# Causal mixing and two gated layers on one core: another fixed order of the engines, and transposes from a doubled copy

## What is computed

```python
w = softmax of weight_gen over its last axis (7 taps, for 8 groups of 24 columns)
out = np.einsum('bshk,bskhg->bshg', w, x_unf)          # causal mixing, 7 taps
x = out.reshape(B * S, 192)
gate = 1.0 / (1.0 + np.exp(-(x @ w_gate)))             # w_gate, w_val: 192 x 1536
y = (gate * (x @ w_val)) @ w_out                       # 1536 x 192
h = y @ w_in                                           # 192 x 2048
P = a[0] + a[1] * h + a[2] * h * h + a[3] * h**3
Q = 1.0 + abs(b[0]) * abs(h) + abs(b[1]) * h * h
out = (P / (Q + 1e-06)) @ w_out2                       # 2048 x 192
```

## Time and profile before

| | |
|---|---|
| median of 3 runs | 1507.46 us (1506.63 to 1507.68) |
| the profiled execution, its own time | 1503.02 us |
| its span | 1501.2 us |
| TensorE clock granted, mean | 0.987 |
| PE matmuls | 7168, busy 93% of the span |
| DVE | busy 86% |
| ACT | busy 70% |
| GpSimd | busy 28% |

### The profile page before, as it was taken

How to read it: one execution, slowest core, us unless ns; L and a number is a source line. 1 busy time by engine, 2 the same in 40 slices (tenths; PEclk the granted TensorE clock), 3 DMA queues, 4 the chain that set the end, 5 groups by cost and what they waited for, 6 DMA issues and landing times.

```text
span 1501.2 us, 18228 instructions
## 1 busy us (share of the span) xinstructions
PE 1402.0 (93%) x7168; PEld 1235.1 (82%) x7168; DVE 1292.8 (86%) x1327; ACT 1044.0 (70%) x1325; POOL 424.9 (28%) x204
## 2 busy tenths in 40 slices
PE   2789999999999999999999999999999999999876
PEld 1678888898888888888888888888888888888766
DVE  6547988989888898988989898898988889888898
ACT  2437777786776777677677767767677777777774
POOL 0650704306060340705125070421607033000000
PEclk9899999999999999999999999999999999999998
DMA  9410000000000000000000000000000000000000
GB/s 198 117 73 30 0 31 11 30 11 30 11 1 30 12 30 11 30 12 1 30 11 30 11 16 15 11 31 12 30 12 0 30 11 1 11 1 11 1 11 11
DMA packets 13102, 36.22 MB, mean 24 GB/s; under 512 B 1240, under 2 KB 6872, under 8 KB 12760
## 3 DMA queue, kind: packets, MB, share of 16 engines
q1 hardware_dynamic: 12952, 35.05, 7.8%
q0 software_dynamic: 64, 0.00, 0.0%
...
## 4 chain that ended last, share of the span: by engine, by line
PE 51%; DVE 33%; ACT 10%; issue 6%; DMA 1%; DVEq 0%; SPq 0%; ACTq 0%
PE ring L280 28%; PE acc L308 21%; DVE work L592 8%; DVE work L604 7%; DVE work L597 4%; ACT work L428 4%; DVE work L578 3%; DVE work L582 3%; DVE work L587 3%; ACT work L423 2%; DVE u L573 2%; ACT L423 1%; ACT work L418 1%; PE ring L335 1%; DVE xt L558 1%
## 5 line engine op out<-in xcount | busy, mean ns | idle before, releaser
L308 PE MATMUL acc<-out_w,work 128*128 128x192 f32 x2048 | 383.7, 331 | 23.1 <-DVE work L604 23.1
L308 PEld LDWEIGHTS acc<-out_w,work 128*128 128x128 f32 x2048 | 347.3, 193 | 43.8 <-DVE work L604 30.4
L280 PE MATMUL ring<-yt,in_w 128*128 128x512 f32 x1280 | 367.9, 417 | 3.1 <-DVE yt L567 3.1
L413 ACT ACTIVATE work<-ring,coef 128x512 f32<-128x512 f32 x256 | 175.0, 683 | 237.9 <-PE ring L280 168.3
L308 PE MATMUL acc<-out_w,u 128*128 128x192 f32 x1536 | 282.3, 327 | 12.6 <-DVE u L573 12.6
L280 PE MATMUL ring<-xt,gate_w 128*128 128x512 f32 x960 | 272.5, 414 | 18.4 <-DVE work L582 13.8
L308 PEld LDWEIGHTS acc<-out_w,u 128*128 128x128 f32 x1536 | 260.3, 190 | 30.2 <-DVE u L573 13.9
L578 DVE TENSOR_TENSOR work<-ring,work 128x512 f32<-128x512 f32 x256 | 175.5, 685 | 126.3 <-ACT work L418 125.8
L280 PEld LDWEIGHTS ring<-yt,in_w 128*128 128x128 f32 x1280 | 236.6, 190 | 42.8 <-issue 3.3
L280 PE MATMUL ring<-xt,val_w 128*128 128x512 f32 x960 | 256.4, 397 | 0.0
L505 POOL TENSOR_TENSOR mixed<-window,mixw 128x768 f32<-128x768 f32 x14 | 21.7, 1550 | 776.0 <-PE ring L340 776.0
...
## 6 DMA issues: line engine op xcount, KB each, us to landing
...
```

What stands on the lines that cost most here:

```text
L280: last = nc.tensor.matmul(dst[:, :], wt[:, c], xs[:, :], start=n == 0, stop=n == 4)
L308: last = nc.tensor.matmul(dst, src[:, n * P:(n + 1) * P], w[:, i, :], start=i == 0 and n % 2 == 0, stop=i == last_i and n % 2 == 1, skip_g ...
L413: nc.scalar.activation(den(n), h[:, :], ACT.Abs, scale=coef[:, 6:7])
```

## The change

- **Transposes.** `mixed` and `ysb` get 256 columns for each 128 tokens, the last 64 a copy of columns 128 to 191. ACT writes it: x_twice is one more copy for each tile (PE now waits for it by s_twice), y_copy becomes two copies. The second bank is then four transposes of columns 128 to 255 in place of eight (L341 of the kernel after). The mixing instructions are the same in number and size, with views of more dimensions.
- **Weights.** The lower 64 rows of each first weight had a high copy in both halves of one tile and a low copy in both halves of another. Now one tile holds the high part in rows 0 to 63 and the low part in rows 64 to 127, and is used for two matmuls in a row, against the high part of x in both halves (xt 2) and the low part in both halves (a fourth tile, xt 3). The number of matmuls of a product stays five. x_low and y_low write 128 rows in place of 64 for their second part, and the split of such a weight's piece writes its low part in 64 rows in place of 128.
- **Order.** PE, ACT and DVE have new orders within a quarter. The lags are the same: B_LAG = 8 counts blocks where 2 counted quarters. X and Y are units of the string. NK is 73, and the last two quarters hold nothing. h_parts and linear are one function, hidden.

The diff, cut to its core (besides it, functions return at once for blocks that don't exist, and mix has views for the wider `mixed`):

```diff
-QUARTER = "21b" "2a1b" "2ab1" "2ab"
+
+
+QUARTER = "12a212abbbXbYa12"
 A_LAG = 1
-X_AT = 10
-Y_AT = 8
+B_LAG = 8
 OFF2 = 5
-B_LAG = 2
...
-        gate_w = [sb(f"gate_w{n}", [P, F1 * P], F32R) for n in range(4)]
-        val_w = [sb(f"val_w{n}", [P, F1 * P], F32R) for n in range(4)]
-        in_w = [sb(f"in_w{n}", [P, F2 * P], F32R) for n in range(4)]
+        gate_w = [sb(f"gate_w{n}", [P, F1 * P], F32R) for n in range(3)]
+        val_w = [sb(f"val_w{n}", [P, F1 * P], F32R) for n in range(3)]
+        in_w = [sb(f"in_w{n}", [P, F2 * P], F32R) for n in range(3)]
...
-        mixed = sb("mixed", [P, J, D])
+        mixed = sb("mixed", [P, J, 2 * P])
...
-        xt = [[sb(f"xt{b}_{n}", [P, T], F32R) for n in range(3)] for b in range(2)]
-        yt = [[sb(f"yt{b}_{n}", [P, T], F32R) for n in range(3)] for b in range(2)]
-        ysb = sb("ysb", [P, J, D])
...
+        xt = [[sb(f"xt{b}_{n}", [P, T], F32R) for n in range(4)] for b in range(2)]
+        yt = [[sb(f"yt{b}_{n}", [P, T], F32R) for n in range(4)] for b in range(2)]
+        ysb = sb("ysb", [P, J, 2 * P])
...
-                passes = [(w[0], src[0]), (w[1], src[0]), (w[0], src[1]), (w[2], src[2]), (w[3], src[2])]
+                passes = [(w[0], src[0]), (w[1], src[0]), (w[0], src[1]), (w[2], src[2]), (w[2], src[3])]
...
-                    dst = bank(u, j, 1)
-                    nc.tensor.transpose(dst[:, n * P:(n + 1) * P], src[:, n, D - P:D], ident[:, :])
-                    last = nc.tensor.transpose(dst[0:DB, n * P:(n + 1) * P], src[:, n, DA:D], ident[:, :])
+                    last = nc.tensor.transpose(bank(u, j, 1)[:, n * P:(n + 1) * P], src[:, n, DA:2 * P], ident[:, :])
                 return last
 
             def x_transposes(j):
-                pe.wait_ge(s_mix, MIXES * (j + 1))
+                pe.wait_ge(s_twice, j + 1)
...
-                m, a, n, b = 3 * k, 3 * k - A_LAG, 4 * (k - OFF2), 4 * (k - OFF2 - B_LAG)
-                for at, u in enumerate(QUARTER):
+                m, a, n, b = 3 * k, 3 * k - A_LAG, 4 * (k - OFF2), 4 * (k - OFF2) - B_LAG
...
+            def x_twice(j):
+                if not 0 <= j < NCH:
+                    return
+                act.wait_ge(s_mix, MIXES * (j + 1))
+                nc.scalar.copy(mixed[:, :, D:2 * P], mixed[:, :, DA:D]).then_inc(s_twice, 1)
...
-                nc.scalar.copy(ysb[:, :, :].rearrange("p (a n) d -> p a (n d)", a=2),
-                               acc1[:, :, 0:2 * D]).then_inc(s_ysb, 1)
+                src = acc1[:, :, 0:2 * D].rearrange("p a (n d) -> p a n d", d=D)
+                dst = ysb[:, :, :].rearrange("p (a n) d -> p a n d", a=2)
+                nc.scalar.copy(dst[:, :, :, 0:D], src)
+                nc.scalar.copy(dst[:, :, :, D:2 * P], src[:, :, :, DA:D]).then_inc(s_ysb, 1)
...
-                one, m = k < 4 * NCH, 3 * k
-                two, n = 0 <= k - OFF2 < 4 * NCH, 4 * (k - OFF2)
-                if two:
-                    h_parts(n)
-                    linear(n)
-                if one:
-                    sigmoid(m)
+                m, n, q = 3 * k, 4 * (k - OFF2), k - OFF2
+                sigmoid(m)
                 if k == 0:
                     split_high(4)
                     split_high(5)
                     exponential(1)
                     split_high(6)
                     split_high(7)
-                if 0 < k < 4 * NCH + 1 and k % 4 == 0:
+                hidden(n)
+                if k % 4 == 0:
                     y_copy(k // 4 - 1)
-                if two:
-                    h_parts(n + 1)
-                    linear(n + 1)
-                if one:
-                    sigmoid(m + 1)
+                if k % 4 == 2:
+                    x_twice((k + 1) // 4 + 1)
+                hidden(n + 1)
+                sigmoid(m + 1)
                 if k == 1:
                     exponential(2)
                 if k in (2, 3):
-                    for p in range(3 * k + 2, 3 * k + 5):
-                        split_high(p)
-                if 0 <= k - OFF2 - 1 < 4 * NCH:
-                    rsqrt(k - OFF2 - 1)
-                if two:
-                    h_parts(n + 2)
-                    linear(n + 2)
-                if 0 < k < 4 * NCH + 1 and k % 4 == 0:
+                    for c in range(3 * k + 2, 3 * k + 5):
+                        split_high(c)
+                rsqrt(q - 1)
+                hidden(n + 2)
+                rsqrt_squared(q - 1)
+                if k % 4 == 3:
+                    x_high(k // 4 + 1)
+                if k % 4 == 0:
                     y_high(k // 4 - 1)
-                if 0 <= k - OFF2 - 1 < 4 * NCH:
-                    rsqrt_squared(k - OFF2 - 1)
-                if one:
-                    sigmoid(m + 2)
-                if k % 4 == 3 and k // 4 + 1 < NCH:
-                    x_high(k // 4 + 1)
-                if two:
-                    h_parts(n + 3)
-                    linear(n + 3)
-                if k >= OFF2 + B_LAG + 3 and (k - OFF2 - B_LAG) % 4 == 3:
-                    z_copy((k - OFF2 - B_LAG) // 4)
+                sigmoid(m + 2)
+                hidden(n + 3)
+                if (k - OFF2) % 4 == 1:
+                    z_copy((k - OFF2 - 1) // 4 - 1)
...
-                nc.vector.tensor_tensor(lo[:, at:at + size], piece[n % BUFFERS][:, 0:size],
-                                        hi[:, at:at + size].bitcast(F32), ALU.subtract).then_inc(s_split, 1)
+                nc.vector.tensor_tensor(lo[rows, at:at + size], piece[n % BUFFERS][rows, 0:size],
+                                        hi[rows, at:at + size].bitcast(F32), ALU.subtract).then_inc(s_split, 1)
...
-                nc.vector.tensor_tensor(dst[2][DB:P, :], bank("X", j, 1)[DB:P, :], dst[2][DB:P, :].bitcast(F32),
+                nc.vector.tensor_tensor(dst[3][:, :], bank("X", j, 1)[:, :], dst[2][:, :].bitcast(F32),
...
-                one, m = k < 4 * NCH, 3 * k
-                two, n = 0 <= k - OFF2 < 4 * NCH, 4 * (k - OFF2)
-
-                p = n // 2 - 2
-                late, due = 0 <= p - 1 < N2 // 2, 0 <= p < N2 // 2
-                if two:
-                    quadratic(n)
-                    cubic(n)
-                if one:
-                    gated(m)
+                m, n, p = 3 * k, 4 * (k - OFF2), 2 * (k - OFF2)
+                gated(m)
                 if k == 0:
                     split_low(4)
                     split_low(5)
@@ -632,46 +657,37 @@
                         soft(step)
                     split_low(6)
                     split_low(7)
-                if late:
-                    reciprocal(p - 1)
-                    quotient(p - 1)
-                if two:
-                    quadratic(n + 1)
-                    cubic(n + 1)
-                    denominator(n // 2)
-                if one:
-                    gated(m + 1)
+                quadratic(n)
+                cubic(n)
+                reciprocal(p - 3)
+                denominator(p - 1)
+                quotient(p - 3)
+                gated(m + 1)
                 if k == 1:
-                    soft(12)
-                    soft(13)
-                    soft(14)
+                    for step in range(12, 15):
+                        soft(step)
                 if k == 2:
-                    soft(15)
-                    soft(16)
-                    soft(17)
+                    for step in range(15, 18):
+                        soft(step)
                 if k in (2, 3):
                     for c in range(3 * k + 2, 3 * k + 5):
                         split_low(c)
-                if two:
-                    quadratic(n + 2)
-                    cubic(n + 2)
-                if 0 < k < 4 * NCH + 1 and k % 4 == 0:
+                quadratic(n + 1)
+                denominator(p)
+                cubic(n + 1)
+                quadratic(n + 2)
+                cubic(n + 2)
+                newton_product(p - 2)
+                if k % 4 == 0:
                     y_low(k // 4 - 1)
-                if due:
-                    newton_product(p)
-                    reciprocal(p)
-                if one:
-                    gated(m + 2)
-                if due:
-                    quotient(p)
-                if k % 4 == 3 and k // 4 + 1 < NCH:
+                if k % 4 == 3:
                     x_low(k // 4 + 1)
-                if two:
-                    quadratic(n + 3)
-                    cubic(n + 3)
-                    denominator(n // 2 + 1)
-                if due:
-                    newton_product(p + 1)
+                reciprocal(p - 2)
+                gated(m + 2)
+                quotient(p - 2)
+                quadratic(n + 3)
+                cubic(n + 3)
+                newton_product(p - 1)
```

79 lines of the change are left out of this document (59 added, 20 removed).

## The result

The kernel after takes 1509.92 us (median of 17 runs, 1508.07 to 1511.6), the kernel before in the same sets of runs 1506.66 (17 runs, 1504.83 to 1509.11). The ratio is 1.0019 with a 95% interval of 1.0011 to 1.0026: slower by 0.2%, small but clear of the noise. I had forecast 1498.6 us, faster with a chance of 0.65. The time is inside the range, but the sign was wrong, and the forecast missed by 11 us.

A forecast was written before the change was run, and what follows sets the result against it. PE bounds quiet quarters, DVE those beside GpSimd's mixing. -13.8 + 2 + 1.5 + 1.5 = -8.8 us on 1503.02 gives 1494.2 profiled; with 4.4 for the runs' median, 1498.6 us. Range for 8 in 10: 1477 to 1515.

The forecast's parts named there:

- What bounds the kernel: PE sets the pace in quiet quarters, DVE while GpSimd mixes; PE waits about 3.4 us in each tile.
- Transposes, -13.8: Four fewer in each of 32 sets, 128 x 0.108 us of PE's work, taken whole: -13.8 us.
- Copies and weights, 0: Extra ACT copies are covered, repeated weights keep their own loads, 128 rows cost DVE as much as 64: 0.
- The quiet quarter, 0: Quarters without mixing: smallest slack in the new order is 1.3 us, so a quarter stays at 20.7 us: 0.
- The order beside GpSimd, +2: During mixing PE waits 3.55 us in a tile where it waited 3.4; over 13 tiles +2 us, bounds -18 to +21.
- The head, +1.5: First quarters: a moved in1 delays DVE's softmax by 2.4 us, a covered wait gives back 0.9: +1.5, 0 to +4.
- The tail, +1.5: Last quarters, DVE the bound: +1.6 over four quarters, +2.4 at the last denominator, -2.4 in quarter 64: +1.5, 0 to +5.
- The smaller slack: Rival: the banks' 1.3 us slack decides, PE waits 5.7 us in a tile, +30 instead of +2, 1526 us; chance 0.17.
- The transposes' gain is not realised: Rival: where DVE sets the pace, waits grow by what PE saves; 1509.5 us, or 1505.6 for Y alone; chance 0.14.
- The order that takes up the surplus: Rival: cubic and quotient ready early beside GpSimd, 1.5 us wait in a tile, 1472 us, half-way 1485; chance 0.17.
- The second load of the same weight: Rival: a weight used by two matmuls in a row loads once, 38 us at most saved, 1460 us; chance 0.02.

The follow-up runs named there:

- two moves on DVE: Against the change: quotient ahead of denominator and cubic ahead of the other denominator while the first layer runs, plus the head's and tail's moves; 1477.51 us.

## Why the prediction was wrong

What follows goes by the steps of the prediction.

**What bounds the kernel: right.** Quiet quarters at PE's own pace, all waits beside GpSimd: the two kernels without mixing have tiles of 84.60 and 85.53 us and no wait.

**Transposes, -13.8: right in size, and not where I put it.** Eight in 0.88 us, and 0.93 us between the two kernels' shortest tiles. But I took them whole, with the waits reckoned apart, as if a shorter set could not change a wait. In the old order the Y sets alone moved it by 1.3 us a tile. In the new order 0.32 us of 0.93 came through where the clock stays up, and on average of the tiles nothing (88.72 and 88.74). Taking the gain whole was a failed step too.

**Copies and weights, 0: nearly.** No wait for x_twice in the middle. In the head I had missed a part: the splits of weights now alternate between 128 and 64 rows, a pair of them takes 1.94 us for 1.81. In the old order with the copy the X transposes of tile 1 start at 94.89 us, where before had 90.08 (but 92.98 and 93.47 in the two kernels with its head, without mixing and with 128 rows). Part of that is chance: the pair of splits at 41.34 took 3.17 us on DVE with GpSimd's first instruction on tile 1 beginning at 41.56, where before it took 1.82, with GpSimd held back to 41.13 by a transfer. The new order with the old copy has 3.16 as well, and the two kernels with before's head 3.17, so this is no part of the copy; the profiled execution of before is the exception. Against those two the copy's price in the old head is 1.4 to 1.9 us; against before itself it would be 4.8. It was not measured by itself.

**The quiet quarter, 0: right**, 671.93 - 651.23 = 20.70 us on PE:

```profile
651.23 1.45 PE L283 MATMUL ring<-xt,gate_w 128*128 128x512 f32 x5
...
671.93 1.45 PE L283 MATMUL ring<-xt,gate_w 128*128 128x512 f32 x5
```

**The order beside GpSimd, +2: this step failed.** The place was right: the early quotient, which out2 wanted 2.2 us before it came (measured 2.3), and its bound for slowed denominators, 3.9 us a tile, was nearer than the 3.55 I took. And the old wait of 3.4 was the wrong yardstick: with the short Y transposes the old order waits 2.4 (86.98 - 84.6). The new order pays 4.14 on average (88.74 - 84.60), 1.8 us a tile more. Against before's 3.32 it is 0.82 in each of 12 tiles, so the term was about +10 us and not +2; these 8 us are most of the 11.3 that the forecast missed by. The profiled executions of the two kernels with the copy are 27.0 us apart (1509.8 - 1482.8), and twelve tiles make 21 of them. In the forecast for the profiled execution a tile was 88.1; at 88.74 twelve tiles make 8 of the 17.4 us that it missed by.

**The head, +1.5: right mechanism, its parts mis-sized.** The moved in1 was given 2.4 us and is worth 4.3, since the wait ahead of it also brought the clock down, and the copy has the part above. The whole is open: quarter 7 starts 8.2 us late between the two profiled executions, but about 3 of these are those of one execution of before. By the medians the tiles (7.7) and the tail (3.0) already make 10.7 of the 11.3 us that the forecast missed by, which leaves little for the head beyond what I had forecast; that is reckoned, not measured.

**The tail, +1.5: too small, inside its bounds (0 to 5).** It is +4.5. The quarters take 15.8 us in place of 15.3, as forecast. The last denominator did what I forecast as well: its rsqrt now makes DVE wait 2.81 us, where my +2.4 on the old 0.30 gives 2.7:

```profile
1494.38 1.23 DVE L621 SCALAR_TENSOR_TENSOR work<-work 128x1024 f32<-128x1024 f32 x1 [2.81 <-ACT work L446]
```

Moving it back gave 3.5. The wait of 2.38 in quarter 64 did go, but it took no time with it. The last tile's quotient is late too, though nothing is mixed any more (DVE had waited 1.90 us for PE and 1.16 for ACT just before); PE waits 2.12 us for it and needs 4.39 (1416.92 - 1412.53) for the 16 passes behind it, at the lower clock again:

```profile
1412.53 4.55 PE L311 MATMUL acc<-out_w,work 128*128 128x192 f32 x16 [2.12 <-DVE work L637]
1416.92 0.60 PE L338 MATMUL ring<-ident,ysb 128*128 128x128 f32 x4
```

**The rivals.** The smaller slack was refuted: it asked for a wait of 5.7 us in a tile, 3.3 were measured with the clock up, and without mixing none. "The transposes' gain is not realised" is what happened, 1505.6 to 1509.5 against 1509.92, and it had a chance of 0.14. Its reason was right for two thirds of the gain: in the new order the wait grew by 0.61 of the 0.93 us that PE no longer does. The clock took the rest. In the old order it was wrong: there the wait shrank. The order that takes up the surplus exists: two moves on DVE away from the change the tiles are 86.6, and that kernel (1477.51) lies between the two times that this rival gave. The second load of the same weight was not saved: 7040 loads, as many as matmuls.

What stays open: why the tile settles at 86.6 with either of the two DVE orders, and how the last 2 us a tile (86.6 - 84.6) could be won (no order with a shorter tile was found); why the clock fell in some tiles and not in others of the same order; and how much of the head's time is the order's, how much the copy's and how much chance.
